# Pairwise carries, three copies and a subtraction on ScalarE, and a new order at the end of each tile

## The chip, the cores and the metric

The kernel runs on one core of one Trainium2 chip. TensorE (PE in the profile) multiplies matrices, VectorE (DVE) and ScalarE (ACT) work elementwise, GpSimd (POOL) helps a little at the end, and SyncE (SP) issues every DMA. The metric is the time of one execution on the device, in microseconds (us), as the median of several runs. Each engine takes its instructions strictly in the order of its own list; a semaphore holds an instruction back until another engine has counted it up, and everything behind it on that engine waits too.

## The reference, cut to what matters

```
mag = np.sqrt(a_re * a_re + a_im * a_im)
scale = np.minimum(mag, 0.999) / (mag + 1e-06)
a_re_n, a_im_n = (a_re * scale, a_im * scale)
for t in range(S):                      # complex decay per channel, outer product added
    new_re = ar * S_re - ai * S_im
    new_im = ar * S_im + ai * S_re
    S_re, S_im = (new_re + einsum('bhd,bhe->bhde', k[t], v[t]), new_im)
    y[t] = einsum('bhd,bhde->bhe', q[t], S_re)
h = x @ w_in                            # x: y as 3072 tokens x 384
x = (np.maximum(h, 0.0) + np.log1p(np.exp(-np.abs(h)))) @ w_out
out = ((x @ w1) * (x @ w2)) @ w3 @ w_out2
```

There are 4 sequences of 768 tokens, 8 heads of 48 channels, 2048 hidden units in the first dense layer and 1024 in the second. All is float32.

## The kernel before, in words

The tokens are cut into 8 tiles of 384; two tiles make a sequence. For each tile the kernel does three things, each one tile or more ahead of the next:

1. **The preparation** (`prep`, on DVE and ACT): the decays are normalised and their running products p over the tile are formed, so that q times p and k divided by p turn the recurrence into plain products. First the squares of the decay (ACT, line 678, `prep_squares`) and their sum (DVE 954, "m2"); then the inverse root as logarithm (ACT 683), exponential (687), and one Newton step: the square of the root (ACT 694, `prep_root_square`) and two DVE instructions (961 and 964, together "newton"); then the scale (970 "scale start", 974 "scale") and the scaled decay (979, "a"). The running product is built by 7 complex products inside runs of 8 tokens ("run"), three copies that collect the ends of the 48 runs of each channel row (998, 1000, "ends"), a scan over those 48 carries with distances 1, 2, 4, 8, 16, 32 ("carry"), and four wide products (1020, 1022, "by") and two sums ("p", 1029 and 1030). A complex product is four DVE instructions (945, 946, 948, 949). Then q (1039), the sum of p's squares (1043, "p2"), its inverse by logarithm and exponential (ACT 712, 715) with a Newton step of two DVE instructions (1049 and 1051, "inverse"), and k divided (1056 "keys", 1061 "keys end"). SP stores q and k to memory and loads them back stacked by head (`store_k`, `stack_k`).
2. **The attention** of tile n+1 in 6 pieces of half a chunk (`scores`, mask on DVE 1145, `outputs`, new state on DVE 1153, output copy on ACT 741 and a DMA into `x1raw`).
3. **The first dense layer** of tile n in 8 steps j: `up(n, j)` makes 256 hidden units, ACT takes abs, exp and log (752, 756, 758, `softplus`), DVE adds relu (1196, `add_relu`: "sum j"), ACT rounds the high part (765, "high j"), DVE subtracts for the low part (1203, `g_low`: "low j"), and `down(n, j)` multiplies on. Each product is three matmuls of high and low parts (1318 to 1320).

A **slot** n is the code of one tile on each engine. PE's slot runs, for j from 0 to 5, `up(n, j+1)`, the scores of piece j of tile n+1, `down(n, j)`, and the outputs of piece j; then at j = 6 `up(n, 7)`, `down(n, 6)`, `up(n+1, 0)`; `down(n, 7)` is done in the next slot behind `up(n+1, 1)`. `up(n, j+1)` overwrites the memory that sum j reads, so it waits for sum j (for `up(n+1, 1)` that is sum 7 of tile n); scores 0 wait for sum 0 of tile n+1; `up(n+1, 0)` waits for both parts of the low half of x1 (DVE 1117). DVE's slot n also holds the preparation of tile n+2, spread over j by three small tables (`before_mask`, `after_mask`, `after_sum`), and at its end the start of the preparation of tile n+3 ("m2", "newton", "scale", "a"). Slots 0 to 4 have both; slot 5 has the preparation of tile 7 and no next one; slots 6 and 7 have none. Tiles 0 and 1 are prepared ahead of slot 0 (the start). An odd tile has no state update in its last two attention pieces, an even one in all, and so slots 1, 3 and 5 (which hold the attention of an even tile) have one update more at j = 4 and 5 than slots 0, 2, 4 and 6.

On ACT the end of a slot stands thus in the code; the squares of tile n+3 stand ahead of high part 6, and they wait for `te_free`, which DVE line 1051 counts up (1104 in the changed kernel):

```
                        softplus(n, j + 1, split, between)
                        if nxt_prep and j == 5:
                            prep_squares(n + 3)
                        g_high(n, j + 1, split)
```

## Time and profile before

| | us |
|---|---|
| median of 3 runs (985.63 to 987.29) | 986.51 |
| the profiled execution's own time | 987.42 |
| its span, first to last instruction | 985.6 |
| start, until scores 0 of slot 0 | 150.84 |
| DVE busy of a slot of 71.31 | 64.23 |
| PE busy of the same slot | 69.19 |

A row of the timeline reads: start, duration, engine, line, operation, output <- inputs, shapes, count, and in brackets how long the engine had been idle before it and what ended that. Durations of neighbours on one engine overlap by about a tenth of a microsecond. In the windows, each engine has its busy time and, behind x, its instructions.

### The profile page before, as it was taken

The numbers are of one execution on the slowest core, as the hardware profiler recorded it, in microseconds if no ns is written. First come the engines' busy times: TensorE is split into PE (matmuls) and PEld (weight loads), VectorE is DVE, ScalarE is ACT, GpSimd is POOL, SyncE is SP. The second block draws the span as 40 slices with busy tenths as digits, with TensorE's granted clock in tenths as the row PEclk, the third lists the DMA queues.
The fourth block names the chain that finished last, engine by engine and source line by source line (L and its number), as shares of the span: only waits on it lengthen the run. The fifth ranks groups of instructions, "written<-read, shape, count | busy, mean of one in ns | idle before, by whom it ended". The sixth has DMA issues, their size and how long they took to land.

```text
span 985.6 us, 14230 instructions
## 1 busy us (share of the span) xinstructions
PE 900.9 (91%) x5298; PEld 802.6 (81%) x5298; DVE 608.7 (62%) x982; ACT 426.5 (43%) x612; POOL 70.1 (7%) x56
## 2 busy tenths in 40 slices
PE   0973838999999999999999999999999999999998
PEld 0543738989989989989889999999888888888887
DVE  5978878989988998898999833355221212121211
ACT  4142263575574584674665654588112120202011
POOL 0000000000000000000000000000222222222221
PEclk9995668999999999999999999999999999999999
DMA  9666066174263382480570460320101010101000
GB/s 336 242 192 192 20 178 149 27 213 123 99 167 97 107 191 67 130 207 26 151 199 13 115 143 13 131 105 26 56 0 65 1 65 1 64 0 64 0 33 32
DMA packets 97877, 99.49 MB, mean 101 GB/s; under 512 B 6928, under 2 KB 88848, under 8 KB 97808
## 3 DMA queue, kind: packets, MB, share of 16 engines
q1 hardware_dynamic: 97808, 98.59, 34.8%
q8 instruction: 40, 0.66, 0.3%
q14 instruction: 29, 0.24, 0.1%
HBM read 63.96 MB, written 29.88 MB: 95 GB/s over the span
## 4 chain that ended last, share of the span: by engine, by line
PE 62%; DVE 22%; ACT 6%; DVEq 5%; issue 3%; DMA 1%; ACTq 1%; SPq 0%
PE ps L1318 7%; PE ps L1320 7%; PE ps L1319 7%; PE ps_p L1318 7%; PE ps_p L1320 7%; PE ps_p L1319 7%; PE ps_ay L1354 3%; DVE sp L1196 2%; DVE an L1022 2%; PE ps_ay L1320 2%; PE ps_ay L1319 2%; PE ps_ay L1318 2%; PE ps_k L1320 2%; PE ps_k L1319 2%; PE ps_k L1318 2%
## 5 line engine op out<-in xcount | busy, mean ns | idle before, releaser
L1318 PE MATMUL ps<-g_h,wo_h 128*128 128x384 f32 x384 | 133.3, 347 | 2.0 <-DVE g_l L1203 2.0
L649 POOL TENSOR_TENSOR abl<-ab,abh 128x512 fp32r<-128x512 f32 x48 | 69.2, 1442 | 908.6 <-DVE abh L1301 908.6
L1320 PE MATMUL ps<-g_h,wo_l 128*128 128x384 f32 x384 | 129.6, 338 | 0.0
L1319 PE MATMUL ps<-g_l,wo_h 128*128 128x384 f32 x384 | 129.3, 337 | 0.0
L1318 PE MATMUL ps_p<-x1h,win_h 128*128 128x384 f32 x336 | 116.8, 348 | 6.1 <-DVE sp L1196 6.1
L1320 PE MATMUL ps_p<-x1h,win_l 128*128 128x384 f32 x336 | 112.7, 335 | 0.0
L1319 PE MATMUL ps_p<-x1l,win_h 128*128 128x384 f32 x336 | 112.5, 335 | 0.0
L1354 PE MATMUL ps_ay<-stq,stk 96*128 96x128 f32 x384 | 56.9, 296 | 39.6 <-DVE am L1145 15.4
L1354 PEld LDWEIGHTS ps_ay<-stq,stk 96*128 96x128 f32 x384 | 53.8, 208 | 41.8 <-issue 26.0
L1292 DVE TENSOR_TENSOR ab<-ps_ay,bc 128x512 f32<-128x512 f32 x24 | 16.6, 692 | 114.6 <-ACT bc L918 114.6
L765 ACT ACTIVATE g_h<-sp 128x768 fp32r<-128x768 f32 (+1 forms) x71 | 55.4, 780 | 65.9 <-DVE sp L1196 65.5
L752 ACT ACTIVATE sp<-ps_p 128x768 f32<-128x768 f32 (+1 forms) x63 | 46.1, 731 | 86.2 <-PE ps_p L1320 86.2
L1292 DVE TENSOR_TENSOR ab<-ps_p,bc 128x512 f32<-128x512 f32 x24 | 16.6, 692 | 102.9 <-ACT bc L918 102.9
L1196 DVE SCALAR_TENSOR_TENSOR sp<-ps_p,sp 128x768 f32<-128x768 f32 (+1 forms) x63 | 54.7, 868 | 35.0 <-ACT sp L758 31.7
L1318 PEld LDWEIGHTS ps<-g_h,wo_h 128*128 128x128 f32 x384 | 72.9, 190 | 3.7 <-DVE g_l L1203 3.6
L1203 DVE TENSOR_TENSOR g_l<-sp,g_h 128x768 fp32r<-128x768 f32 (+1 forms) x71 | 62.4, 878 | 19.2 <-ACT g_h L765 12.6
L1319 PEld LDWEIGHTS ps<-g_l,wo_h 128*128 128x128 f32 x384 | 72.9, 190 | 0.0
L1320 PEld LDWEIGHTS ps<-g_h,wo_l 128*128 128x128 f32 x384 | 72.6, 189 | 0.0
L1318 PEld LDWEIGHTS ps_p<-x1h,win_h 128*128 128x128 f32 x336 | 63.2, 188 | 9.7 <-DVE sp L1196 9.3
L918 ACT ACTIVATE bc<-ps_k 128x512 f32<-128x512 f32 x24 | 14.4, 598 | 123.6 <-PE ps_k L1320 123.6
L918 ACT ACTIVATE bc<-ps_p 128x512 f32<-128x512 f32 x24 | 14.4, 598 | 118.1 <-PE ps_p L1320 118.1
L1319 PEld LDWEIGHTS ps_p<-x1l,win_h 128*128 128x128 f32 x336 | 63.2, 188 | 0.0
(160 smaller groups left out, 1993.6 us busy)
## 6 DMA issues: line engine op xcount, KB each, us to landing
qk_scr<-tt SPq DMA_DIRECT2D x16, 576.0 KB, 5.1
stq<-qk_scr SPq DMA_DIRECT2D x48, 192.0 KB, 4.8
qk_scr<-pp SPq DMA_DIRECT2D x16, 576.0 KB, 4.0
stk<-qk_scr SPq DMA_DIRECT2D x48, 192.0 KB, 4.5
an<-in_a_re SPq DMA_DIRECT2D x8, 576.0 KB, 3.9
an<-in_a_im SPq DMA_DIRECT2D x8, 576.0 KB, 5.3
qk<-in_q SPq DMA_DIRECT2D x8, 576.0 KB, 7.6
qk<-in_k SPq DMA_DIRECT2D x8, 576.0 KB, 8.9
```

The source lines that it names most:

```text
L649: tensor_tensor(abl[:, m % AR, :], ab[:, m % 2, :], abh[:, m % AR, :].bitcast(F32), ALU.subtract).then_inc(ab_lo, 1)
L752: act(buf, ps_u[j][:, us, 0:T], ACT.Abs)
L765: act(g_h[:, j % GR, us, :], sp[:, j % 2, us, :], ACT.Copy).then_inc(g_hi, us.stop - us.start)
L918: act(bc[:, m % 2, :], ps_ab[m % 2][1], ACT.Copy).then_inc(b_ev, 1)
L1022: ve.tensor_tensor(runs[:, c], runs[:, c], carry_of(1), ALU.mult)
L1196: ve.scalar_tensor_tensor(out=buf, in0=ps_u[j][:, us, 0:T], scalar=0.0, in1=buf, op0=ALU.max, op1=ALU.add)\
L1203: ve.tensor_tensor(g_l[:, j % GR, us, :], sp[:, j % 2, us, :], g_h[:, j % GR, us, :].bitcast(F32), ALU.subtract).then_inc(g_lo, us.stop - ...
L1292: ve.tensor_tensor(ab[:, m % 2, :], ps_ab[m % 2][0], bc[:, m % 2, :], ALU.mult).then_inc(ab_mul, 1)
L1318: mm(o, wh, xh, start=start, stop=False)
L1319: mm(o, wh, xl, start=False, stop=False)
L1320: return mm(o, wl, xh, start=False, stop=stop)
L1354: last = mm(ps_a[:, h4, :], stk[0:D2, h, cs], stq[0:D2, h, cs], start=True, stop=True)
```

## The change

- **Carries by pairs.** The 48 carries of a row are first multiplied in pairs ("carry in"), the 24 pairs are scanned with distances 1, 2, 4, 8, 16, and the results are multiplied back into the odd places ("carry out"): 7 complex products where there were 6, of about half the width.
- **ACT instead of DVE.** The three copies of the ends go to ACT (`prep_ends`, behind the new semaphore `runs_made`; DVE then waits for `ends_out`). In the middle of a slot they stand between the abs and the exp of step 3. The scale is written as min(root, 1/0.999) times (root - 1e6), and ACT makes the difference (`prep_root_less`, between abs and exp of step 0 of the next tile, behind `prep_root_made`; DVE's "scale" waits for `prep_less`). "scale start" is gone.
- **Order.** In the tables the ends and the whole carry work stand behind mask 2. New state 4 stands ahead of p2. Sum 6 stands between the halves of "inverse"; low part 6 stands ahead of m2; "keys end" is cut in two, each half followed by a part of the low half of x1; newton's halves stand behind sum 7, with low part 7 between them. On ACT the square of the root moves behind `softplus` 7. SP stores each half of k as it is done; in the start, piece 6 of the weights is loaded later and some low parts of the weights are made later.

```diff
-                wait(prep_k, m + 1)
                 if not first:
                     for c in range(NCH):
                         wait(k_rd[c], 32 * m)
                 for i in range(2):
+                    wait(prep_k, 2 * m + i + 1)
                     eng.dma_start(c_p(qk_scr[2 + i]), by_g(pp[:, i, :])).then_inc(k_wr, 16)
...
-            for i in range(3, 7):
+            for i in range(3, 6):
                 load_piece(i)
...
                 stack_k(0, c)
+            load_piece(6)
             load_qk(1)
...
+            def prep_ends(m):
+                carries = gp[:, :, :].rearrange("p c (g r) -> p c g r", g=G)
+                ends = an[:, :, :].rearrange("p c (g k i r) -> p c g k i r", g=G, i=RUN, r=CR)
+                most = (NCH - 1) * CR
+                eng.wait_ge(runs_made, m + 1)
+                for c in range(2):
+                    act(carries[:, c, :, 1:1 + most].rearrange("p g (k r) -> p g k r", r=CR),
+                        ends[:, c, :, 0:NCH - 1, RUN - 1, :], ACT.Copy)
+                act(carries[:, :, :, 1 + most:NR], ends[:, :, :, NCH - 1, RUN - 1, 0:CR - 1], ACT.Copy).then_inc(ends_out, 1)
+
+            def prep_root_less(m):
+                eng.wait_ge(prep_root_made, m + 1)
+                act(te[:, 0, :], te[:, 1, :], ACT.Copy, bias=-1e6).then_inc(prep_less, 1)
+
...
+                            if has_prep and j == 2:
+                                prep_ends(n + 2)
...
                     elif j == NP1 - 2:
                         if nxt_prep:
                             prep_log(n + 3)
+                        if nxt:
+                            y_loaded(n + 1, 0)
+                            x1_high(n + 1, 0)
+                        if nxt_prep:
                             prep_root(n + 3)
                         if nxt:
-                            for part in range(2):
-                                y_loaded(n + 1, part)
-                                x1_high(n + 1, part)
+                            y_loaded(n + 1, 1)
+                            x1_high(n + 1, 1)
+                        softplus(n, j + 1, split)
                         if nxt_prep:
                             prep_root_square(n + 3)
-                        softplus(n, j + 1, split)
                         g_high(n, j + 1, split)
                     elif nxt:
-                        softplus(n + 1, 0, False)
+
+                        def less():
+                            if nxt_prep:
+                                prep_root_less(n + 3)
+
+                        softplus(n + 1, 0, False, less)
                         g_high(n + 1, 0, False)
...
-            def prep_newton(m):
+            def prep_newton_start(m):
 
                 eng.wait_ge(prep_rs, m + 1)
                 eng.drain()
                 ve.scalar_tensor_tensor(out=tr[:, :], in0=te[:, 0, :], scalar=-0.5, in1=tt[:, 0, :],
                                         op0=ALU.mult, op1=ALU.mult)
                 eng.drain()
+
+            def prep_newton_end(m):
                 ve.scalar_tensor_tensor(out=te[:, 1, :], in0=tr[:, :], scalar=1.5, in1=te[:, 1, :],
-                                        op0=ALU.add, op1=ALU.mult)
-                eng.drain()
-
-
-            def prep_scale_start(m):
-                ve.tensor_scalar(tr[:, :], te[:, 1, :], 0.999, 1.0, ALU.mult, ALU.min)
-                eng.drain()
+                                        op0=ALU.add, op1=ALU.mult).then_inc(prep_root_made, 1)
+                eng.drain()
+
 
             def prep_scale(m):
-                ve.scalar_tensor_tensor(out=tr[:, :], in0=te[:, 1, :], scalar=-1e6, in1=tr[:, :],
-                                        op0=ALU.add, op1=ALU.mult)
+                eng.wait_ge(prep_less, m + 1)
+                ve.scalar_tensor_tensor(out=tr[:, :], in0=te[:, 1, :], scalar=1.0 / 0.999, in1=te[:, 0, :],
+                                        op0=ALU.min, op1=ALU.mult)
                 eng.drain()
 
             def prep_a(m, c):
-                ve.scalar_tensor_tensor(out=an[:, c, :], in0=an[:, c, :], scalar=-1e-6, in1=tr[:, :], op0=ALU.mult, op1=ALU.mult)
+                ve.scalar_tensor_tensor(out=an[:, c, :], in0=an[:, c, :], scalar=-0.999e-6, in1=tr[:, :], op0=ALU.mult, op1=ALU.mult)
                 eng.drain()
...
+                if i == RUN - 1:
+                    last.then_inc(runs_made, 1)
+
+            def prep_carry_start(m, even):
                 if even:
                     ve.memset(carries[:, 0, :, 0:1], 1.0)
                     ve.memset(carries[:, 1, :, 0:1], 0.0)
                 else:
                     ve.tensor_copy(carries[:, :, :, 0:1], car[:, :, :].unsqueeze(3))
-                ends = an[:, :, :].rearrange("p c (g k i r) -> p c g k i r", g=G, i=RUN, r=CR)
-                most = (NCH - 1) * CR
-                for c in range(2):
-                    ve.tensor_copy(carries[:, c, :, 1:1 + most].rearrange("p g (k r) -> p g k r", r=CR),
-                                   ends[:, c, :, 0:NCH - 1, RUN - 1, :])
-                ve.tensor_copy(carries[:, :, :, 1 + most:NR], ends[:, :, :, NCH - 1, RUN - 1, 0:CR - 1])
-                eng.drain()
+                eng.wait_ge(ends_out, m + 1)
+                eng.drain()
+
+
+            def prep_carry_in():
+                t = gp[:, :, :].rearrange("p c (a l) -> p c a l", l=2)
+                n = GC * CR // 2
...
+                cmul(t[:, 0, :, 1], t[:, 1, :, 1], t[:, :, :, 0],
+                     t[:, 0:1, :, 1].to_broadcast([P, 2, n]), t[:, 1:2, :, 1].to_broadcast([P, 2, n]), m1, m2)
 
             def prep_carry(s_):
 
-                w = NR - s_
+                w = NPAIR - s_
...
-                cmul(carries[:, 0, :, s_:], carries[:, 1, :, s_:], carries[:, :, :, s_:],
-                     carries[:, 0:1, :, 0:w].to_broadcast([P, 2, G, w]), carries[:, 1:2, :, 0:w].to_broadcast([P, 2, G, w]),
...
+                cmul(pairs[:, 0, :, s_:], pairs[:, 1, :, s_:], pairs[:, :, :, s_:],
+                     pairs[:, 0:1, :, 0:w].to_broadcast([P, 2, G, w]), pairs[:, 1:2, :, 0:w].to_broadcast([P, 2, G, w]),
                      m1, m2)
+
+            def prep_carry_out():
+                v = gp[:, :, :].rearrange("p c (g m l) -> p c g m l", g=G, l=2)[:, :, :, 1:, 0]
+                w = NPAIR - 1
...
+                done = pairs[:, :, :, 0:w]
+                cmul(v[:, 0], v[:, 1], v, done[:, 0:1].to_broadcast([P, 2, G, w]), done[:, 1:2].to_broadcast([P, 2, G, w]), m1, m2)
...
-            def prep_inv_newton(m):
+            def prep_inv_start(m):
 
                 eng.wait_ge(prep_inv, m + 1)
                 ve.tensor_tensor(tr[:, :], te[:, 0, :], te[:, 1, :], ALU.mult)
                 eng.drain()
+
+            def prep_inv_end(m):
                 ve.scalar_tensor_tensor(out=tr[:, :], in0=tr[:, :], scalar=2.0, in1=te[:, 1, :],
                                         op0=ALU.subtract, op1=ALU.mult).then_inc(te_free, 1)
                 eng.drain()
@@ -1057,9 +1110,8 @@
...
-            def prep_keys_end(m):
-                ve.tensor_tensor(pp[:, :, :], pp[:, :, :], tr[:, :].unsqueeze(1).to_broadcast([P, 2, GT]), ALU.mult)\
-                    .then_inc(prep_k, 1)
+            def prep_keys_end(m, i):
+                ve.tensor_tensor(pp[:, i, :], pp[:, i, :], tr[:, :], ALU.mult).then_inc(prep_k, 1)
...
-            before_mask = {0: steps("a", 1), 1: steps("run", 3, 4), 2: steps("run", 7) + ["ends"] + steps("carry", 1),
-                           3: steps("carry", 8, 16, 32), 4: by[3:] + ["p"], 5: []}
-            after_mask = {0: steps("run", 1), 1: steps("run", 5), 2: steps("carry", 2), 3: by[:2], 4: [("q", 0)], 5: ["inverse"]}
-            after_sum = {0: steps("run", 2), 1: steps("run", 6), 2: steps("carry", 4), 3: by[2:3], 4: [("q", 1), "p2"], 5: ["keys"]}
+            before_mask = {0: steps("a", 1), 1: steps("run", 3, 4), 2: steps("run", 7),
+                           3: steps("carry", 4, 8, 16) + ["carry out"], 4: by[3:] + ["p"], 5: []}
+            after_mask = {0: steps("run", 1), 1: steps("run", 5), 2: ["ends", "carry in"], 3: by[:2], 4: [("q", 0)], 5: ["inverse start"]}
+            after_sum = {0: steps("run", 2), 1: steps("run", 6), 2: steps("carry", 1, 2), 3: by[2:3], 4: [("q", 1)], 5: ["inverse end", "keys"]}
...
-                    if att and 1 <= j <= NG:
+                    if att and 1 <= j <= NG and j != 5:
                         new_state(n + 1, j - 1)
                     if has_prep and j < 6:
                         prep(n + 2, even, before_mask[j])
@@ -1219,10 +1287,6 @@
                         mask_scores(n + 1, j)
                     if has_prep and j < 6:
                         prep(n + 2, even, after_mask[j])
-                    if j == 6 and nxt:
-                        x1_low(n + 1)
-                    if nxt_prep and j == 6:
-                        prep(n + 3, not even, ["newton"])
                     if j < NP1 - 1:
                         add_relu(n, j + 1, split)
                     elif nxt:
@@ -1231,14 +1295,23 @@
                         add_relu(n + 1, 0, False)
                     if has_prep and j < 6:
                         prep(n + 2, even, after_sum[j])
-                    if nxt_prep and j == 5:
-                        prep(n + 3, not even, ["m2"])
+                    if att and j == 4:
+                        new_state(n + 1, 4)
+                        if has_prep:
+                            prep(n + 2, even, ["p2"])
                     if nxt_prep and j == 6:
-                        prep(n + 3, not even, ["scale start"])
+                        prep(n + 3, not even, ["newton start"])
                     if j < NP1 - 1:
                         g_low(n, j + 1, split)
-                        if has_prep and j == 5:
-                            prep(n + 2, even, ["keys end"])
+                        if nxt_prep and j == 5:
+                            prep(n + 3, not even, ["m2"])
+                        if nxt and j == 5:
+                            for part in range(2):
+                                if has_prep:
+                                    prep(n + 2, even, steps("keys end", part))
+                                x1_low(n + 1, (part,))
+                        if nxt_prep and j == 6:
+                            prep(n + 3, not even, ["newton end"])
                     elif nxt:
                         if nxt_prep:
                             prep(n + 3, not even, steps("a", 0))
```

Two places show how rows move. **DVE, end of slot 1, the inverse** (te, tr and pp are the preparation's, sp and g the dense layer's, x1l the low half of x1). Before:

```order
L1049 TENSOR_TENSOR tr<-te 128x1152 [waits prep_inv]
L1051 SCALAR_TENSOR_TENSOR tr<-tr,te 128x1152
L1196 SCALAR_TENSOR_TENSOR sp<-ps_p,sp 128x768 [waits sp_log]
L1056 SCALAR_TENSOR_TENSOR tr<-qk,tr 128x1152
L954 TENSOR_TENSOR te<-te 128x1152 [waits prep_sq]
L1203 TENSOR_TENSOR g_l<-sp,g_h 128x768 [waits g_hi]
L1061 TENSOR_TENSOR pp<-pp,tr 128x2304
L1153 TENSOR_TENSOR state<-state,ps_k 96x192 [waits yz_mm]
L1117 TENSOR_TENSOR x1l<-x1raw,x1h 128x3x256 [waits x1_hi]
L1117 TENSOR_TENSOR x1l<-x1raw,x1h 128x3x128 [waits x1_hi]
```

and in the changed kernel:

```order
L1100 TENSOR_TENSOR tr<-te 128x1152 [waits prep_inv]
L1263 SCALAR_TENSOR_TENSOR sp<-ps_p,sp 128x768 [waits sp_log]
L1104 SCALAR_TENSOR_TENSOR tr<-tr,te 128x1152
L1109 SCALAR_TENSOR_TENSOR tr<-qk,tr 128x1152
L1270 TENSOR_TENSOR g_l<-sp,g_h 128x768 [waits g_hi]
L992 TENSOR_TENSOR te<-te 128x1152 [waits prep_sq]
L1114 TENSOR_TENSOR pp<-pp,tr 128x1152
L1182 TENSOR_TENSOR x1l<-x1raw,x1h 128x3x256 [waits x1_hi]
L1114 TENSOR_TENSOR pp<-pp,tr 128x1152
L1182 TENSOR_TENSOR x1l<-x1raw,x1h 128x3x128 [waits x1_hi]
```

Sum 6 (the row sp<-ps_p,sp) has moved from behind both rows of the inverse to between them, m2 (te<-te behind prep_sq) from ahead of the low part to behind it, and the 2304 wide product is now two of 1152. **DVE, the next rows, the root.** Before:

```order
L961 SCALAR_TENSOR_TENSOR tr<-te,tt 128x1152 [waits prep_rs]
L964 SCALAR_TENSOR_TENSOR te<-tr,te 128x1152
L1196 SCALAR_TENSOR_TENSOR sp<-ps_p,sp 128x768 [waits sp_log]
L970 TENSOR_SCALAR tr<-te 128x1152
L1203 TENSOR_TENSOR g_l<-sp,g_h 128x768 [waits g_hi]
L974 SCALAR_TENSOR_TENSOR tr<-te,tr 128x1152
L1196 SCALAR_TENSOR_TENSOR sp<-ps_ay,sp 128x768 [waits sp_log]
```

and in the changed kernel:

```order
L1263 SCALAR_TENSOR_TENSOR sp<-ps_p,sp 128x768 [waits sp_log]
L999 SCALAR_TENSOR_TENSOR tr<-te,tt 128x1152 [waits prep_rs]
L1270 TENSOR_TENSOR g_l<-sp,g_h 128x768 [waits g_hi]
L1004 SCALAR_TENSOR_TENSOR te<-tr,te 128x1152
L1011 SCALAR_TENSOR_TENSOR tr<-te 128x1152 [waits prep_less]
L1263 SCALAR_TENSOR_TENSOR sp<-ps_ay,sp 128x768 [waits sp_log]
```

The two rows of the Newton step stood ahead of sum 7 and are now behind it, with low part 7 between them; the last row is sum 0 of the next tile, and the row ahead of it waits for ACT. **ACT at the same place**, from the last row of `softplus` 7. Before:

```order
L758 ACTIVATE sp<-sp 128x768
L765 ACTIVATE g_h<-sp 128x768 [waits p_sum,g_free]
L752 ACTIVATE sp<-ps_ay 128x768 [waits p_mm,g_lo]
L756 ACTIVATE sp<-sp 128x768
L758 ACTIVATE sp<-sp 128x768
L765 ACTIVATE g_h<-sp 128x768 [waits p_sum,g_free]
```

and in the changed kernel:

```order
L779 ACTIVATE sp<-sp 128x768
L700 ACTIVATE tt<-te 128x1152 [waits q_wr]
L786 ACTIVATE g_h<-sp 128x768 [waits p_sum,g_free]
L773 ACTIVATE sp<-ps_ay 128x768 [waits p_mm,g_lo]
L719 ACTIVATE te<-te 128x1152 [waits prep_root_made]
L777 ACTIVATE sp<-sp 128x768
```

The square of the root (tt<-te) has come behind the logarithm of step 7, and the row that waits for prep_root_made stands between the abs and the exp of step 0.

## Rows read from the trace of the kernel before

**Rows 1.** The page, the chain that ended last by engine
```profile
PE 62%; DVE 22%; ACT 6%; DVEq 5%; issue 3%; DMA 1%; ACTq 1%; SPq 0%
```

**Rows 2.** Windows of slots 1 and 5: length, busy time of PE, PEld, DVE, ACT
```profile
217.85:289.16 71.31, 69.19 (x489) 65.33 (x489) 64.23 (x105) 44.22 (x63) 0.00 (x0) 1.00 0.46 125
501.64:570.17 68.53, 68.31 (x488) 65.36 (x489) 60.10 (x101) 39.39 (x57) 0.00 (x0) 1.00 0.44 113
```

**Rows 3.** Timeline of PE in slot 1 and at slot 2's start
```profile
257.77 0.42 PE L1318 MATMUL ps_p<-x1h,win_h 128*128 128x384 f32 x1
...
271.15 0.57 PE L1354 MATMUL ps_ay<-stq,stk 96*128 96x128 f32 x3 [0.60 <-DVE state L1153]
...
281.11 0.45 PE L1318 MATMUL ps<-g_h,wo_h 128*128 128x384 f32 x1 [0.31 <-DVE g_l L1203]
...
285.17 0.44 PE L1318 MATMUL ps_ay<-x1h,win_h 128*128 128x384 f32 x1 [0.65 <-DVE x1l L1117]
...
289.16 0.44 PE L1318 MATMUL ps_p<-x1h,win_h 128*128 128x384 f32 x1 [0.56 <-DVE sp L1196]
...
295.53 0.39 PE L1354 MATMUL ps_ay<-stq,stk 96*128 96x128 f32 x2
```

**Rows 4.** Timeline of DVE at the end of slot 1
```profile
274.68 1.36 DVE L1051 SCALAR_TENSOR_TENSOR tr<-tr,te 128x1152 f32<-128x1152 f32 x1
276.20 0.96 DVE L1196 SCALAR_TENSOR_TENSOR sp<-ps_p,sp 128x768 f32<-128x768 f32 x1 [0.16 <-issue]
...
278.57 1.36 DVE L954 TENSOR_TENSOR te<-te 128x1152 f32<-128x1152 f32 x1
280.09 0.96 DVE L1203 TENSOR_TENSOR g_l<-sp,g_h 128x768 fp32r<-128x768 f32 x1 [0.16 <-issue]
280.97 2.55 DVE L1061 TENSOR_TENSOR pp<-pp,tr 128x2304 f32<-128x2304 f32 x1
...
283.70 1.42 DVE L1117 TENSOR_TENSOR x1l<-x1raw,x1h 128x768 fp32r<-128x768 f32 x2
```

**Rows 5.** Timeline of ACT at the end of slot 1
```profile
274.13 0.85 ACT L758 ACTIVATE sp<-sp 128x768 f32<-128x768 f32 x1
276.13 1.17 ACT L678 ACTIVATE te<-an 128x1152 f32<-128x1152 f32 x1 [1.15 <-DVE tr L1051]
...
278.45 0.83 ACT L765 ACTIVATE g_h<-sp 128x768 fp32r<-128x768 f32 x1
...
283.76 1.15 ACT L694 ACTIVATE tt<-te 128x1152 f32<-128x1152 f32 x1
...
291.74 0.85 ACT L758 ACTIVATE sp<-sp 128x768 f32<-128x768 f32 x1
```

**Rows 6.** Groups of DVE by line and form: busy us and mean ns of one
```profile
L970 DVE TENSOR_SCALAR tr<-te 128x1152 f32<-128x1152 f32 x8 | 6.0, 754 | 0.2
L945 DVE TENSOR_TENSOR ms<-gp 128x282 f32<-128x282 f32 x8 | 3.6, 454 | 0.6
L945 DVE TENSOR_TENSOR ms<-gp 128x96 f32<-128x96 f32 x8 | 2.1, 258 | 0.5
L998 DVE COPY gp<-an 128x96 f32<-128x96 f32 x16 | 2.8, 217 | 0.0
```

**Rows 7.** Timelines of DVE and PE in the start
```profile
72.61 1.36 DVE L961 SCALAR_TENSOR_TENSOR tr<-te,tt 128x1152 f32<-128x1152 f32 x1 [3.76 <-ACT tt L694]
...
150.84 0.55 PE L1354 MATMUL ps_ay<-stq,stk 96*128 96x128 f32 x1 [13.04 <-DMA vt<-in_v]
```

**Rows 8.** Timeline of DVE, sums 3 and 4 of slot 1
```profile
246.09 0.96 DVE L1196 SCALAR_TENSOR_TENSOR sp<-ps_p,sp 128x768 f32<-128x768 f32 x1
...
256.19 0.95 DVE L1196 SCALAR_TENSOR_TENSOR sp<-ps_p,sp 128x768 f32<-128x768 f32 x1
```

**Rows 9.** Groups of ACT by line and form, the new state's copy
```profile
L744 ACT ACTIVATE state<-ps_k 96x192 f32<-96x192 f32 x6 | 1.9, 317 | 0.0
```

**Rows 10.** Timeline of SP, the loads of k behind slot 1's end
```profile
288.20 1.86 SPq L419 DMA_DIRECT2D stk<-qk_scr  x4
```

More of the change, by code:

```diff
@@ L31 @@
 CR = CT // RUN
+NPAIR = NR // 2
 GC = G * NCH
@@ L1069, in prep @@
                     elif piece == "newton":
-                        prep_newton(m)
-                    elif piece == "scale start":
-                        prep_scale_start(m)
+                        prep_newton_start(m)
+                        prep_newton_end(m)
+                    elif piece == "newton start":
+                        prep_newton_start(m)
+                    elif piece == "newton end":
+                        prep_newton_end(m)
                     elif piece == "scale":
@@ L1077, in prep @@
                     elif piece == "ends":
-                        prep_carry_start(even)
+                        prep_carry_start(m, even)
                     elif piece == "p":
@@ L1157, in _ @@
             raw_low(0)
-            prep(0, True, ["newton", "scale start", "scale"] + steps("a", 0, 1) + steps("run", 1, 2))
+            prep(0, True, ["newton"])
             raw_low(1)
+            prep(0, True, ["scale"] + steps("a", 0, 1) + steps("run", 1, 2))
             prep(0, True, steps("run", 3, 4, 5, 6, 7))
             raw_low(2)
-            prep(0, True, ["ends"] + steps("carry", 1, 2, 4))
+            prep(0, True, ["ends", "carry in"] + steps("carry", 1, 2, 4, 8, 16) + ["carry out"] + by + ["p", ("q", 0), ("q", 1), "p2", "inverse", "keys"] + steps("keys end", 0, 1), first=True)
+            prep(1, False, ["m2"])
             raw_low(3)
-            prep(0, True, steps("carry", 8, 16, 32) + by + ["p", ("q", 0), ("q", 1), "p2", "inverse", "keys", "keys end"], first=True)
-            prep(1, False, ["m2", "newton", "scale start", "scale"] + steps("a", 0, 1))
+            prep(1, False, ["newton", "scale"] + steps("a", 0, 1))
             for i in range(4, 7):
@@ L1182, in _ @@
             x1_low(0)
-            prep(1, False, ["p2", "inverse", "keys", "keys end"])
+            prep(1, False, ["p2", "inverse", "keys"] + steps("keys end", 0, 1))
             prep(2, True, ["m2"])
```

50 lines of the change are left out of this document (38 added, 12 removed).

## The prediction

> **What bounds the kernel now.** I read the chain that ended last first: 62% of it is TensorE, 22% VectorE [rows 1], so the two take turns. Then the windows of the slots: slot 1 lasts 71.31 us with DVE busy for 64.2 and the TensorE clock granted in full (1.00, 2.4 GHz), and slot 5, which has the preparation of tile 7 but not the start of another, lasts 68.53 [rows 2]. Slot 5 does the same PE work as slot 1, so some 2.8 us of slot 1 are waits. The timeline of PE shows where: 0.60 for new state 4 at 271.15, 0.31 for low part 6 at 281.11, 0.65 for the low half of x1 at 285.17, 0.56 for sum 7 at 289.16 [rows 3], 2.12 together; the remaining 0.66 is a restart of 0.2 to 0.3 beside each. All four are releases by DVE, and three stand in the last 10 us of the tile. There the order on DVE and ACT decides, and the timelines of both are what the rest is worked out from [rows 4, 5].
>
> **The gains on DVE.** "scale start" goes: 0.75 [rows 6], 0.83 with the drain behind it. Three copies of 0.22 [rows 6] overlapped go to ACT: 0.5. Carries: a 282 wide product costs 0.45 and a 96 wide one 0.26 [rows 6], so a complex product is some 1.49 us at the full width and 0.91 where its products are 96 wide. On that line the old six come to 7.87 (1.49, 1.49, 1.43, 1.35, 1.20, 0.91) and the new seven (144, 138, 132, 120, 96, 48, 138 wide) to 6.8: 1.07 less. The extra half of "keys end" costs 0.1. Together 2.3 us a tile. If the strided access of pairs cost as much as it saves, this would be 1.2.
>
> **In the start** these are on the path: 0.83 + 0.5 + 1.07 for tile 0, and 1.7 for low part 3 of the weights (1536 wide; the 2304 wide product takes 2.55 [rows 4]), which moves into DVE's wait of 3.76 for the root of tile 1 [rows 7]: 4.1. For tile 1 DVE has nothing to do between the Newton step and "scale" while ACT makes the difference, 1.16 as its other 1152 wide passes [rows 5] and two hops, 1.3 against 0.83: 0.5 lost; then 0.5 + 1.07 in tile 1's carries, and some 0.5 as the first half of k is stored earlier, ahead of the wait of 13.04 at 150.84 [rows 7]. Sum: 5.6; I take -5, with 3.5 (the transfers hide part) to 6.5 as its ends.
>
> **The middle of a slot.** Behind mask 2 DVE now waits for ACT's three copies, and they stand between abs and exp of step 3, so sum 3 (246.09 [rows 8]) is late by them. The trace has no such copy; the ends are 0.22 for each (DVE's own [rows 6]) and 0.32 (ACT, 192 wide [rows 9]), less 0.1 of overlap each: I take 0.5 for all, nearer the second. And behind sum 3 stand 5.75 us of pair carries (2.06 and 3.69) where 4.89 stood (1.43 and 3.46), since carry 1 and 2 used to be done around the mask. So sum 4 comes 0.5 + 0.9 = 1.3 later: it ends at 258.45 and not 257.14 [rows 8]. up 5 on PE starts at 257.77 without idle time [rows 3], so it now waits 0.7 and restarts: +0.8 to 0.9. In slots 1, 3 and 5 the wait at 271.15 (0.60 + 0.27) goes in return, as new state 4 moves ahead of p2; in slots 0, 2 and 4 there is no such wait to win.
>
> The Trainium skill, page "VectorE: DVE Perf Modes", section on the TRN2 errata of SBUF sources, gives a ScalarE instruction from SBUF a fixed 224 cycles plus one per element at 1.2 GHz, 0.27 us for a 96 wide copy, paid by each small instruction anew. The trace's 0.32 for 192 wide lies near it; by it, taken without overlap, the copies are 0.8 and the sum at the end would be 1.8 higher.
>
> **The inverse at a tile's end** (clock of slot 1). DVE comes to p2 1.3 + 0.27 late (new state 4 is now ahead of it), ACT's inverse and log 6 follow: log 6 started at 274.13 and ended at 274.98 [rows 5]; now it ends at 276.3. Sum 6 stands ahead of the second half of the inverse, and that half releases `te_free`. Before, this half ended at 276.04, ahead of sum 6 at 276.20 [rows 4], and ACT's squares started at 276.13 [rows 5]. Now sum 6 runs 276.4 to 277.3 and the half ends at 278.65. Behind the squares on ACT stands high part 6: 278.45 - 276.13 = 2.32 later [rows 5], so from 281.1 to 281.9; low part 6 ends at 282.9, not 281.05 [rows 4]: **+1.85**. Moving m2 behind it saved nothing, since the squares are what is late.
>
> **x1.** Behind low part 6 now come m2 (1.43), half of k (1.27), x1 low 0, half of k, x1 low 1. Before, it was 4.05 to the end of x1 low at 285.1 [rows 4]. On ACT the log of tile n+3 (1.17) waits for m2 and stands ahead of the first x1 high (768 wide, 0.8 as high part 6), so x1 low 0 starts at 286.25, and 0.87 + 1.27 + 0.5 later x1 low ends at 288.95. up(n+1, 0) goes from 285.17 [rows 3] to 289.05: **+3.9**.
>
> **Sum 7** no longer stands behind newton. Log 7 ends at 290.4, sum 7 at 291.4, and up(n+1, 0) is at work until 292.2 (3.15 us, half of the 6.37 that two such blocks take from 289.16 to 295.53 [rows 3]): the wait of 0.56 with its restart is gone, up(n+1, 1) comes at 292.2 for 289.16: **+3.05**.
>
> **The root and "less".** Now one chain leads from log 7 (290.4) to sum 0: square on ACT 1.1, first half on DVE 1.4, low part 7 0.9, second half 1.4, difference on ACT 1.25, exp 0.95, log 0.85, sum 0 1.0; it ends at 299.25. Before, newton was done ahead of sum 7, log 0 ended at 292.59 [rows 5], and scores 0 followed at their natural place, 295.53. Now their natural place is 298.5 and they wait 0.75; high and low part 0 follow sum 0 (high 0.85, low 0.95), so `down(n+1, 0)` waits 1.0 more. With two restarts: +1.9. PE is then **+5.0** late in slots 1 and 3, and, for want of the state's wait, +5.7 in slots 0, 2 and 4. So each of five tile ends costs 5.0 or 5.7, which is 27.1. Slot 5 has no squares: 0.9 in the middle, about 0.5 at low part 6, 1 at x1 low, less its state's wait: +2.
>
> **Sum:** 27.1 + 2 - 5 = +24. The profiled execution lay 1.8 us above its span of 985.6, at 987.42, and 0.9 above the median of 986.51; the span would be 1009.7, the median 1010.5. Work behind slot 7 is untouched. With 4 to 6 us for an end (4 if the middle delays nothing: then the second half ends 1 us sooner and all follows), 1 to 3 for slot 5, and -3.5 to -6.5 in the start, the likeliest case runs from 1001 to 1016.
>
> **The rivals.**
> - *The waits vanish, as less work would have it* (faster). For it: DVE is busy 64 of 71 us and 2.3 go; each of five slots could lose its 2.8, that is 14, and the start 5: 967 to 972. It decides if log 6 ends no later than the first half of the inverse; but before, the first half started at 273.25 (1.43 ahead of 274.68 [rows 4]) and log 6 ended at 274.98 [rows 5], so sum 6 becomes ready 0.3 behind the end of the first half at best, and its own 0.9 is in the squares' way in any case: 1.2. Chance 0.06.
> - *Half the price*: DVE and ACT catch up, so that an end costs 2: 10 + 1 - 6 = +5, 991. Against it: no link of the root's chain above can run beside another. Chance 0.12, and 0.03 that gains and losses cancel within 0.2%.
> - *Late k holds the scores too.* Before, the last of k was ready at 283.52 [rows 4], its loads were issued 4.7 us later, at 288.20 [rows 10], and scores 0 came 7.3 us behind them. Now k is ready at 288.4, its loads are issued at 293.1, and scores 0 come at 299.3, 6.2 us behind. If 7.3 is what the loads need, each end costs 1.1 to 1.5 more: 1017. Chance 0.09.
> - The likeliest case: 0.70.
>
> **How the numbers follow.** A difference under 0.2% (2 us) can't be told from none. The range leaves out the faster rival, the even one and about half of the two cases beside the likeliest, 0.19 in all: 996 to 1018. Faster 0.06, same 0.03, slower 0.91.
>
> **What would show it.** In the trace after: DVE's wait ahead of sum 6 for the log, and ACT's ahead of the squares; PE's wait for low part 6 near 2 us and for x1 low near 2; a new wait of ACT for the second half of newton ahead of the difference (1.5 to 2 us), and PE's for sum 0. up(n+1, 1) no longer waits for sum 7. Slots of 75 to 76 us. Scores 0 of slot 0 near 146. Wrong if slots last under 71, which would mean that the squares start within 0.5 us of their old place.

## The result and the profile after

The changed kernel takes **1016.07 us** (median of 4, 1012.99 to 1017.44), the kernel before 986.73 (985.63 to 987.29) beside it: ratio **1.0294**, 95% interval 1.0272 to 1.0315. The forecast was 1010.5, in a range of 996 to 1018.

The page of the changed kernel, its chain by engine ([rows 1] before):

```profile
PE 54%; DVE 19%; ACT 12%; DVEq 7%; issue 4%; ACTq 2%; DMA 1%; SPq 0%
```

ACT's share has doubled. Next the four windows from `up(n, 0)` to `up(n+1, 0)` for n = 1 to 4; each runs from near the end of slot n-1 to near the end of slot n (columns as in [rows 2]; the number behind POOL is the granted clock). The kernel before took 71.32, 70.58, 71.29 and 70.25 between the same places, with DVE busy for 64.2 to 64.3 at a clock of 1.00:

```profile
216.20:292.81 76.61, 72.59 (x488) 68.54 (x489) 61.90 (x105) 45.73 (x68) 0.00 (x0) 0.96 0.43 117
292.81:369.35 76.54, 69.83 (x481) 65.85 (x481) 62.36 (x108) 44.53 (x64) 0.00 (x0) 0.98 0.42 117
369.35:445.91 76.56, 69.50 (x488) 65.55 (x489) 61.99 (x105) 45.61 (x68) 0.00 (x0) 1.00 0.43 117
445.91:523.99 78.08, 69.84 (x481) 65.86 (x481) 62.42 (x108) 44.61 (x64) 0.00 (x0) 0.98 0.42 115
```

DVE has 1.9 to 2.3 us less to do (2.3 was forecast), and yet the stretches are longer by 5.3, 6.0, 5.3 and 7.8. PE at the end of slot 1 shows where (beside [rows 3]):

```profile
286.88 0.44 PE L1391 MATMUL ps<-g_h,wo_h 128*128 128x384 f32 x1 [2.06 <-DVE g_l L1270]
292.81 0.44 PE L1391 MATMUL ps_ay<-x1h,win_h 128*128 128x384 f32 x1 [0.96 <-DVE x1l L1182]
303.80 1.13 PE L1427 MATMUL ps_ay<-stq,stk 96*128 96x128 f32 x8 [1.34 <-DVE sp L1263]
305.86 0.44 PE L1391 MATMUL ps<-g_h,wo_h 128*128 128x384 f32 x1 [0.60 <-ACT x1raw L833]
```

The 0.60 is put down to x1raw, but low part 0, which `down` needs too, ends only at 305.8 (304.85 + 0.96, DVE's last row below). Sum 7 is no longer waited for. DVE at the same place, beside [rows 4]:

```profile
277.32 1.36 DVE L1100 TENSOR_TENSOR tr<-te 128x1152 f32<-128x1152 f32 x1
280.31 0.96 DVE L1263 SCALAR_TENSOR_TENSOR sp<-ps_p,sp 128x768 f32<-128x768 f32 x1 [1.62 <-ACT sp L779]
281.18 1.35 DVE L1104 SCALAR_TENSOR_TENSOR tr<-tr,te 128x1152 f32<-128x1152 f32 x1
...
285.86 0.96 DVE L1270 TENSOR_TENSOR g_l<-sp,g_h 128x768 fp32r<-128x768 f32 x1 [1.89 <-ACT g_h L786]
...
292.20 0.55 DVE L1182 TENSOR_TENSOR x1l<-x1raw,x1h 128x384 fp32r<-128x384 f32 x1
...
294.54 0.96 DVE L1263 SCALAR_TENSOR_TENSOR sp<-ps_p,sp 128x768 f32<-128x768 f32 x1 [1.53 <-ACT sp L779]
...
297.98 1.35 DVE L1004 SCALAR_TENSOR_TENSOR te<-tr,te 128x1152 f32<-128x1152 f32 x1
300.57 1.36 DVE L1011 SCALAR_TENSOR_TENSOR tr<-te 128x1152 f32<-128x1152 f32 x1 [1.24 <-ACT te L719]
302.48 0.96 DVE L1263 SCALAR_TENSOR_TENSOR sp<-ps_ay,sp 128x768 f32<-128x768 f32 x1 [0.56 <-ACT sp L779]
...
304.85 0.96 DVE L1270 TENSOR_TENSOR g_l<-sp,g_h 128x768 fp32r<-128x768 f32 x1
```

and ACT, beside [rows 5]:

```profile
282.62 1.17 ACT L684 ACTIVATE te<-an 128x1152 f32<-128x1152 f32 x1 [2.42 <-DVE tr L1104]
...
288.12 1.16 ACT L689 ACTIVATE te<-te 128x1152 f32<-128x1152 f32 x1 [2.10 <-DVE te L992]
...
299.37 1.17 ACT L719 ACTIVATE te<-te 128x1152 f32<-128x1152 f32 x1 [2.20 <-DVE te L1004]
```

The two engines now wait for each other in turn: DVE 1.62 for log 6 with the inverse half done, ACT 2.42 for the other half, DVE 1.89 for high part 6 behind the squares, ACT 2.10 for m2 behind low part 6, DVE 1.53 for log 7, ACT 2.20 for the second half of newton, DVE 1.24 for the difference. Before, DVE had no wait over 0.40 between mask 5 and sum 0 of the next tile, and ACT waited 1.15 ahead of the squares and 0.42 ahead of the logarithm.

The start gained 2.5 and not 5. Scores 0 of slot 0, at 150.84 in [rows 7], now begin at 148.35:

```profile
148.35 2.05 PE L1427 MATMUL ps_ay<-stq,stk 96*128 96x128 f32 x8 [12.34 <-DMA vt<-in_v]
```

### The profile page after: what moved, and what is told of

The parts are those of the page before. It is cut to its first block, busy times and chain, and to the rows that moved or that the text cites. A ratio compares the mean times of both kernels' runs of the same rounds, so it can differ in the third digit from the quotient of the medians.

```text
span 1015.7 us, 14278 instructions
## 1 busy us (share of the span) xinstructions
PE 915.1 (90%) x5298; PEld 814.2 (80%) x5298; DVE 591.6 (58%) x990; ACT 439.3 (43%) x644; POOL 70.0 (7%) x56
## 4 chain that ended last, share of the span: by engine, by line
PE 54%; DVE 19%; ACT 12%; DVEq 7%; issue 4%; ACTq 2%; DMA 1%; SPq 0%
PE ps L1391 6%; PE ps L1393 6%; PE ps L1392 6%; PE ps_p L1391 6%; PE ps_p L1393 6%; PE ps_p L1392 6%; DVE sp L1263 3%; PE ps_ay L1427 2%; ACT sp L779 2%; ACT sp L777 2%; DVE an L1073 2%; PE ps_ay L1391 2%; PE ps_ay L1393 2%; PE ps_ay L1392 2%; DVE g_l L1270 2%
## 5 line engine op out<-in xcount | busy, mean ns | idle before, releaser
L1391 PE MATMUL ps<-g_h,wo_h 128*128 128x384 f32 x384 | 135.9, 354 | 13.7 <-DVE g_l L1270 10.9
```

The costliest lines, as they stand in the source:

```text
L1391: mm(o, wh, xh, start=start, stop=False)
```

## The experiments

Theory T: the order at a tile's end costs the time, since instructions that release the other engine stand behind waits. Rival R: ACT's added load, the stride of the pairs, or the clock. The kernel before, run beside each, had 986.3 to 986.9. Prices are differences of medians; each median has an uncertainty of 1 to 2 us, as the intervals of the ratios show.

**Undoing the end's order, piece by piece.** `inverse_whole`, in DVE's tables:

```diff
-5: ["inverse start"]}  ...  5: ["inverse end", "keys"]}
+5: ["inverse"]}        ...  5: ["keys"]}
```

> The changed kernel, with both halves of the inverse ahead of sum 6 again, nothing else. Theory T (the end of a tile is late because instructions that release others stand behind waits in DVE's order): the second half of the inverse ends some 2.4 us earlier than in the changed kernel, so ACT's squares and high part 6 come 2.4 earlier and the wait of PE for low part 6 (2.06 in slot 1) is gone; each of five tile ends gets 2.0 to 2.4 back and slot 5 0.3 to 0.9, which gives 1003 to 1006. Rival R (the added load of ACT, the strided access of the pairs and the lower clock after waits are the cause, not the order): 1014 to 1016, PE's wait only moves on to the low half of x1.

Measured: **1002.70** (ratio 1.0166, 1.0149 to 1.0183), 13.4 less, 0.3 beyond the range of T and far from R. PE no longer waits for low part 6. As R had it, part of the wait comes back at x1, but only part:

```profile
287.14 0.44 PE L1391 MATMUL ps_ay<-x1h,win_h 128*128 128x384 f32 x1 [2.44 <-DVE x1l L1182]
298.13 1.13 PE L1427 MATMUL ps_ay<-stq,stk 96*128 96x128 f32 x8 [1.35 <-DVE sp L1263]
```

This is the second of five ends: `up(n+1, 0)` comes 3.2 earlier than in the changed kernel at the first (212.97 for 216.20) and 5.7 earlier here, of which 0.25 comes from the start. The traced execution was the slowest of its four (1006.62), so its rows show less than the 13.4.

`root_back`:

```diff
-softplus(n, j + 1, split)      # ACT: square behind it
-prep_root_square(n + 3)
+prep_root_square(n + 3)
+softplus(n, j + 1, split)
...
+prep(n + 3, not even, ["newton"])      # DVE: ahead of sum 7, its halves gone behind it
 add_relu(n, j + 1, split)
```

> The changed kernel, with both halves of the Newton step ahead of sum 7 and ACT's square of the root ahead of softplus 7 again. T: the chain square, half, low part, half, difference is broken up; ACT's difference no longer waits (2.20 in slot 1), sum 0 comes 1.1 to 2 earlier and PE's waits of 1.34 and 0.60 for sum 0 and low part 0 go; sum 7 comes up to 1.4 later and PE waits for it again, some 0.5 to 0.9. Each end gets 1 to 1.4 back: 1009 to 1011. R: no change, 1015 to 1017.

Measured: **1010.05** (1.0247, 1.0230 to 1.0264). PE waits 0.86 for sum 7 (at 291.92) and no longer for sum 0. It is 6.0 less, inside the range of T. (The rows are of its fastest execution, 1007.52, in which the start ran 3 us shorter at a higher clock; see the last section.)

`keys_back`, which also puts the first high part of x1 behind the root's exponential again on ACT:

```diff
-g_low(n, j + 1, split)
 prep(n + 3, not even, ["m2"])
-for part in range(2):
-    prep(n + 2, even, steps("keys end", part)); x1_low(n + 1, (part,))
+g_low(n, j + 1, split)
+prep(n + 2, even, steps("keys end", 0, 1)); x1_low(n + 1)
```

> The changed kernel with only the third piece of the end's order as before: m2 ahead of low part 6, both halves of k ahead of both parts of x1's low half, the first x1 high part behind the root's exponential. It tells whether the three pieces of the order add up: the inverse alone gave 13.4 us back, the root 6.0, all together 25.6, which leaves 6.2 for this piece. If they add (each piece delays another link): 1008 to 1011, with low part 6 some 0.6 later and x1's low half 1.4 earlier. Rival: what m2 costs ahead of low part 6 eats the gain at x1, 1014 to 1017, and the 6.2 were an interaction of the other two.

Measured: **1005.90** (1.0191, 1.0172 to 1.0209), 10.2 less, more than either side had it.

```profile
284.27 0.44 PE L1389 MATMUL ps<-g_h,wo_h 128*128 128x384 f32 x1 [2.77 <-DVE g_l L1269]
```

```profile
283.13 1.16 ACT L689 ACTIVATE te<-te 128x1152 f32<-128x1152 f32 x1 [0.43 <-DVE te L991]
```

PE's wait for low part 6 has grown (2.77 for 2.06), but for x1 and sum 7 PE waits no more than 0.3, since m2, and with it ACT's logarithm and root, no longer stand behind the low part: ACT's wait ahead of that logarithm is 0.43 and not 2.10. The forecast had said that moving m2 behind low part 6 "saved nothing"; in fact it cost. How the 10.2 are shared between m2, the halves of k and the place of x1's high part was not measured.

`end_back`, all three pieces:

> The changed kernel with the whole order of a tile's end as before: inverse ahead of sum 6, m2 ahead of low part 6, both halves of k ahead of x1's low half, newton ahead of sum 7, the square ahead of softplus 7, x1's high parts behind the root. Pair carries, ACT's copies and ACT's difference, new state 4 ahead of p2, and the start stay changed. T: the slots fall from 76.5 to 70.5 to 71.5 us, and the start's gain of 2.5 stays: 983 to 989. R (load of ACT, strides and clock): above 1005.

Measured: **990.46** (1.0040, 1.0028 to 1.0053). The order of the end alone costs 25.6 us. The pieces come to 13.4 + 6.0 + 10.2 = 29.6; whether they really overlap by 4 is open, since all three prices rest on the same median of four executions, 1012.99 to 1017.44 (by the ratios the pieces come to 27.4 and the whole to 25.1). As the cause of the 25.6, ACT's added work and the stride of the pairs are out, for both are still in this kernel. The clock is not separated by it, since its falls go with the waits; the trace puts 1.5 us on them (last section). The time lies 1.5 above the range of T; two stretches, through slots 1 and 2, last 71.78 and 72.37, for 71.32 and 70.58 before, and the next run shows that this is the middle's work.

**The middle.** `middle_back` is end_back with

```diff
-2: steps("run", 7), ... 2: ["ends", "carry in"], ... 2: steps("carry", 1, 2)
+2: steps("run", 7) + ["ends", "carry in"], ... 2: steps("carry", 1), ... 2: steps("carry", 2)
```

and the three copies of the slots on DVE; `copies_dve` has these copies on DVE too but keeps the changed places. (In the start both leave the copies on ACT.)

> The kernel end_back (whole end as before) with the middle as before too: in the slots the three copies on DVE again, copies and carry in ahead of mask 2, carry 1 behind it, carry 2 behind sum 3; ACT's copies stay in the start alone. It prices the middle. Theory: PE's waits of 0.55 and 0.90 in slots 0, 2, 4 and of 0.53 in slots 1, 3, 5 go, each with some 0.2 of restart: 1.8 and 0.8 a slot, 5 to 8 us in all, 983 to 985. Rival: these waits only come back at the tile's end, since DVE is as full as before: 988 to 990.

> The kernel end_back (whole end as before, middle changed, 990.46) with the three copies of the ends in the slots on DVE, at the same place behind mask 2; all carries stay behind mask 2. Together with middle_back (984.0) it splits the price of the middle, 6.4 us: into that of ACT's copies, which I put at 0.5 a slot, and that of the place of the carry work behind the mask, 0.86. Theory: DVE waits 0.39 for ACT's copies in end_back and would spend about 0.5 on its own, so the copies' engine is worth nothing here and the place is all of it: 989 to 991.5. Rival: ACT's copies, which delay its exp and logarithm of step 3, are at least half of it: 985 to 988.

Measured: **984.00** (0.9977, 0.9967 to 0.9987) and **988.19** (1.0020, 1.0010 to 1.0029). So the middle costs 6.4 to 6.5: ACT's copies 2.3, with an uncertainty nearly as large, and the place of the carry work 4.2. I had expected no gain from the engine of the copies, which was wrong, and also the rival's "at least half": it is a third, near the shares of the forecast's own terms (0.5 and 0.86). DVE in the changed kernel, slot 1:

```profile
247.50 0.69 DVE L1210 TENSOR_TENSOR am<-ps_ay,mask 128x512 f32<-128x512 f32 x1 [1.57 <-PE ps_k L1430]
...
248.60 0.31 DVE L982 TENSOR_TENSOR ms<-gp 128x144 f32<-128x144 f32 x1 [0.33 <-ACT gp L715]
...
250.45 0.96 DVE L1263 SCALAR_TENSOR_TENSOR sp<-ps_p,sp 128x768 f32<-128x768 f32 x1 [0.86 <-ACT sp L779]
```

DVE sits idle for 1.57 ahead of mask 2 while the work that could fill the time stands behind it, and sum 3 waits 0.86 for ACT's logarithm. That the copies put this logarithm off shows between the two kernels: sum 3 starts 2.95 behind mask 2 in end_back (244.47) and 2.44 in copies_dve (241.99), where its wait is 0.25.

**Parts of the change and new moves, on the kernel before.** `pairs_start`, which also loads piece 6 of the weights later:

```diff
-after_mask 2: carry 2; after_sum 2: carry 4; before_mask 3: carry 8, 16, 32
+before_mask 2: ... "carry in"; after_mask 2: carry 1; after_sum 2: carry 2; before_mask 3: carry 4, 8, 16, "carry out"
...
-            raw_low(3)                    # start, ahead of carry 8
+            prep(1, False, ["m2"])
+            raw_low(3)
```

> The kernel before with two parts of the change alone: the carries by pairs (with the copies of the ends still on DVE, and the order of carries around masks and sums as before), and in the start low part 3 of the weights behind the sum of squares of tile 1 and piece 6 loaded later. T: DVE has 1.07 us less a tile, the start gains 1 to 3 and the slots 0 to 0.7 each: 980 to 985. R (the stride of the pairs costs as much as their half width saves): 985 to 987 or above.

Measured: **982.58** (0.9963, 0.9949 to 0.9977), faster than before and in the range of T. Its windows:

```profile
209.72:280.78 71.06, 69.14 (x488) 65.28 (x488) 62.99 (x108) 44.14 (x64) 0.00 (x0) 1.00 0.47 127
280.78:351.01 70.23, 67.84 (x480) 64.13 (x480) 63.06 (x110) 42.88 (x60) 0.00 (x0) 1.00 0.47 126
```

DVE is busy 1.24 less than before a slot, but a slot wins only 0.3; of the 5.1 by which the span is shorter, 3.6 are the start (scores 0 at 147.23). The stride of the pairs costs nothing that shows: a product of 144 elements takes 0.31 (the row at 248.60 above), as on the line through the two widths of [rows 6].

`carry_early` puts carry 2 into DVE's wait ahead of sum 3:

```diff
-2: steps("carry", 1), ... 2: steps("carry", 2)
+2: steps("carry", 1, 2), ... 2: []
```

> The kernel pairs_start with one move: the pair carry of distance 2 stands ahead of sum 3 (behind mask 2) and no longer behind it. DVE waits there 0.77 to 0.87 for ACT's logarithm, and from there to sum 7 it has no idle time in slots 0, 2 and 4. Theory: the carry (1.0) fills this wait, sum 3 comes 0.2 later, all behind it 0.8 earlier, and PE's waits at the tile's end (0.56, 0.49, 0.45, 0.59 in slots 0, 2, 4; 0.66, 0.59 in slots 1, 3) shrink by up to 0.8 a slot: 979 to 981. Rival: the waits at the end hang on ACT's chain (logarithm, squares, root) and not on DVE: 982 to 983; or sum 3 holds PE up: above 983.

Measured: **983.35** (0.9971, 0.9958 to 0.9983): no gain over pairs_start, as its rival had it. DVE's idle time moved on, and the next new state came to hold up scores (0.61 and 0.31 at 267.65 and 409.17).

`x1_early` adds to it, with k in halves and, on DVE, both low parts of x1 between the halves; on ACT:

```diff
 prep_log(n + 3)
+y_loaded, x1_high (both parts)
 prep_root(n + 3)
-y_loaded, x1_high (both parts)
```

> The kernel carry_early with x1's low half earlier, at a place where it delays nothing: on ACT both x1 high parts stand between the root's logarithm and exponential, on DVE both x1 low parts between the halves of k, and SP stores each half of k as it is done. The newton step and sum 7 keep their places. Theory: PE's wait for x1's low half goes (0.45 to 0.66 and a restart, in five slots), but the wait for sum 7 grows by as much as PE is then early, unless the carry move has made sum 7 earlier: 976 to 980. Rival: sum 7 takes the whole gain back, the time of carry_early within 1.

Measured: **990.14** (1.0053, 1.0033 to 1.0073), 6.8 more than carry_early, worse than the rival. On ACT:

```profile
350.36 0.53 ACT L724 ACTIVATE x1h<-x1raw 128x384 fp32r<-128x384 f32 x1 [1.25 <-DMA x1raw<-ys]
350.96 1.17 ACT L689 ACTIVATE te<-te 128x1152 f32<-128x1152 f32 x1
```

The second part of x1raw had not arrived; ACT waited 1.25 for the transfer with the root behind it, and PE waits 1.76 to 2.49 for sum 7 at the ends of slots 0 to 4. I had not looked at when the transfer lands.

**The start.** `loads_early`, on pairs_start:

```diff
 store_q(1)
-store_k(1)
 wait(yz_mm, NG)
-for c in range(NCH): stack_q(1, c); stack_k(1, c); load_v(1, c)
+for c in range(NCH): stack_q(1, c); load_v(1, c)
+store_k(1)                       # each half of k as it is done
+for c in range(NCH): stack_k(1, c)
```

> The kernel pairs_start (982.58) with another order on SP at the end of the start: the loads of stacked q and of v for tile 1 stand ahead of the store of k, not behind it between the loads of stacked k, and each half of k is stored as it is done. PE's scores 0 of slot 0 wait 11.96 us there, until 147.23, for the load of v that was issued at 143.28, while q was ready at 124.4 and v from the beginning. Theory: scores 0 then wait for the load of k issued at 142.42 or a little before, which lands some 3.4 later, so they start 1.4 to 2 us earlier: 980.5 to 981.5. Rival: the loads share the DMA engines with the store of k and delay it by as much, 982 to 983.

Measured: **986.30** (0.9992, 0.9981 to 1.0002), 3.7 above pairs_start (2.9 by the ratios) and above the rival's 982 to 983 too. SP's queue: k was stored at 138.56 and stacked k could be loaded only at 146.47, 7.9 us later; in pairs_start it was 136.92 and 142.42, 5.5 us:

```profile
138.56 0.91 SPq L405 DMA_DIRECT2D qk_scr<-pp  x2
146.47 2.90 SPq L420 DMA_DIRECT2D stk<-qk_scr  x6
```

Scores 0 start at 150.75 for 147.23. Of the 4.05 by which stacked k is loaded later, 0.8 stood ahead of it on DVE (k's last product ends 0.8 later, in a start that ran at a lower clock for PE), 0.9 is SP's list, where the early loads are issued until the store can be, and 2.4 is the store itself: its two transfers landed 6.5 and 7.5 us behind their issue, for 3.0 and 5.1. The likely reason is that the loads just ahead move at the same time; which transfers held which was not traced.

`masks_early` (with loads_early) and `masks_alone` (on pairs_start) put mask 0 of tile 0 ahead of this work for tile 1:

```diff
+mask_scores(0, 0)
-for i in range(4, 7): prep(1, False, steps("run", i - 3)); raw_low(i)
-prep(1, False, steps("run", 4))
-mask_scores(0, 0)
+prep(1, False, steps("run", 1)); raw_low(4)      # runs 2 to 7, low parts 5 and 6: between the masks
```

> loads_early with another order on DVE in the start: mask 0 of tile 0 ahead of the runs 1 to 4 of tile 1 and of the low parts of three pieces of the weights, which are spread between the masks. In pairs_start DVE waits 2.81, 1.43 and 1.27 for PE ahead of masks 1, 2 and 3 and 0.97 at the last state, while PE waits 12.23 for mask 0. Theory: the start is bound by DVE's work plus these waits; they go, and scores 0 of slot 0 come 4 to 5 us earlier: 976 to 977.5. Rival: the time goes into other waits (ACT's copies of k behind the high part of a late piece, the transfers), or into a lower clock for PE: 979 or above.

> The kernel pairs_start with the early masks alone: SP's order as in pairs_start, k of tile 1 stored in one piece of work and the loads of q and v between those of k. In masks_early (980.78) and loads_early (986.3) the store of k took 7.8 and 7.9 us from its first issue to the first load of stacked k, where pairs_start took 5.5, so the two parts pull against each other. Theory: the masks are worth 5.5 (980.78 against 986.3) whatever SP does, and the early loads cost 3.7: 982.58 - 5.5 = 977.1, 976.5 to 978.5. Rival: both reach the same limit of the transfers, 980 to 981.

Measured: **980.78** (0.9944, 0.9930 to 0.9958) and **978.81** (0.9922, 0.9908 to 0.9935). masks_early missed its theory (976 to 977.5) and lies where its rival had it. The masks are worth 5.5 beside the early loads and 3.8 without them (4.7 and 4.0 by the ratios), which is too near to tell whether the two parts add; masks_alone lies 0.3 outside the range given. The store of k behaves as in loads_early and pairs_start: its transfers land after 6.4 and 6.6 with the early loads, 3.0 and 5.1 without. masks_alone is the fastest kernel, 0.78% under the kernel before; its scores 0 start at 144.24.

## Why the prediction was right, and where it was not

- **Sign and mechanism**: right. The rows that it named are there: DVE's wait ahead of sum 6 (1.62), ACT's ahead of the squares (2.42), PE's for low part 6 (2.06), ACT's for the second half of newton (2.20), PE's for sum 0 (1.34); `up(n+1, 1)` waits no more. Undoing the order gave 25.6 us back, so this is shown, not only argued.
- **The number alone would have misled.** 1016.07 is 5.6 above the forecast, just past the 1016 that ended its likeliest case, and nearest to the 1017 of a rival, late k. That rival did not happen: the two loads of k that scores 0 of slot 2 need were issued at 295.31 and 295.7 and landed 3.1 and 3.5 us later, by 299.3, while sum 0, which released the scores, ended at 303.44.
- **An end**: nearly as worked out, link by link. Counted from `up` 3 of slot 1 (238.94 before, 242.85 after), sum 4 starts 1.3 later (1.3 was forecast), low part 6 ends 1.86 later (+1.85), `up(2, 0)` comes 3.73 later (+3.9), `up(2, 1)` 2.99 (+3.05) and `up` 2 of slot 2 5.30 (+5.0). Only the last link, from log 7 to sum 0 and to `down`, was 0.4 too small. From `up` 2 of one slot to that of the next, slots 0 to 5 last longer by 6.3, 5.3, 6.0, 6.8, 5.9 and 2.0, which is 32.3 for a forecast of 29.1 (5.7 and 5.0 in turn, and 2). Of the 3.2, 1.5 is the lower clock near 459 (below), in the 6.8, and the rest 0.3 to 0.6 an end.
- **"Moving m2 behind it saved nothing"** was too kind: keys_back shows that the logarithm, x1 and sum 7 stand behind m2. The forecast did have this cost, as part of "+3.9" at x1, but not that undoing it was worth 10 us.
- **The middle**: the copies were put at 0.5 on ACT, and in end_back the exp starts 1.09 behind the copy of k and not 0.57 (copies_dve), 0.52 more; the 0.8 that the forecast named as the other price is not what the trace shows. (A copy 90 wide takes 0.27 by itself, but the three overlap; the row of 0.32 that the forecast compared with reads from PSUM, while the copies read from SBUF.) PE's wait of 0.53 to 0.55 for sum 4 is there in slots 0 to 4. But in slots 0, 2 and 4 a second one of 0.9 follows, which the sum did not have. In the changed kernel little of it shows (6.0 more in slot 2, for 5.7); in end_back, with the end as before, the stretch through slot 2 is 1.8 longer than before and the one through slot 1 only 0.5.
- **The start, "-5"**: the term with the largest miss. It was 2.5 in the profiled execution (scores 0 at 148.35 for 150.84). The instructions were costed rightly: mask 0 came at 88.16 for 91.64, 3.5 earlier. Of this 2.1 was lost in tile 0's attention, where DVE waits 2.93 and 1.50 for PE (0.83 and nothing before), and 1.1 came on top behind it:

```profile
101.56 0.69 DVE L1210 TENSOR_TENSOR am<-ps_ay,mask 128x512 f32<-128x512 f32 x1 [2.93 <-PE ps_k L1430]
```

  The sum took DVE to be the path there; PE at half clock is as long. Luck has a part in this term either way: the seven traced kernels with this start have scores 0 at 145.28 to 148.35, a gain of 2.5 to 5.6, and the one traced execution of the kernel before had a clock of 0.58 and 0.71 where the changed kernel had 0.50 (from 96 to 108 and from 108 to 120).
- **The total**: 30.1 us of span against 24.1. 2.5 of the 6 are the start, 1.5 the clock in slot 4, and the rest the ends. All three misses go the same way; the range held the time, but with 2 us to spare, and its upper part was there for a case that did not occur.

## What to carry to other kernels

Two engines that release each other need their order read together: a step cut in halves, with a wait between them, puts that wait in front of whatever the second half releases, and here some 2 us less work a tile came out as 5 to 8 us more time. Fill an idle stretch with work that is ready ahead of it, and not by moving a releasing instruction behind a wait; and before an instruction is moved forward, look up when its transfer lands and what its own transfers share. Price such edits one at a time, since 25.6 us was made of pieces of 13.4, 10.2 and 6.0, and the second of these had been taken for nothing.
